# Experts' raw weights loaded into the place of their low part, and two places for a tile's inner rows

## What is computed

```python
def _moe2_ref(x, w_gate, w_output_gate, w1, w2) -> np.ndarray:
    logits = x @ w_gate
    e_idx = np.argmax(logits, axis=1)
    ...
    for e in range(E):
        mask = e_idx == e
        ...
        h = np.maximum(x[mask] @ w1[e], 0.0)
        ye = h @ w2[e]
        out[mask] = gate_w[mask, None] * eom[mask, e, None] * ye
```

## Time and profile before

| | |
|---|---|
| median of three runs | 1172.2 us (1169.95, 1172.2, 1597.25) |
| the profiled execution | 1167.76 us, its span 1166.0 us |
| mean granted TensorE clock | 0.988 |
| TensorE matmuls busy | 1127.7 us, 97% of the span |
| VectorE, ScalarE, GpSimd busy | 639.4, 466.8, 76.8 us |
| DMA over the span | 131.36 MB, mean 113 GB/s |

### The profile page before, as it was taken

The page is one execution under the profiler, slowest core; times in us unless marked ns, Lnnn a source line. Parts: engine busy times, 40 slices in busy tenths (PEclk is TensorE's granted clock), DMA queues, the critical chain, the costliest instruction groups (busy, mean ns, idle before and its releaser), DMA issues.

```text
span 1166.0 us, 20895 instructions
## 1 busy us (share of the span) xinstructions
PE 1127.7 (97%) x6358; PEld 886.0 (76%) x6359; DVE 639.4 (55%) x1247; ACT 466.8 (40%) x780; POOL 76.8 (7%) x96
## 2 busy tenths in 40 slices
PE   9999999999999999999999988989999999979995
PEld 7777777777777777777778977777888888858884
DVE  6675654655646556556564347557464435556632
ACT  4554434443444444434544351435342223344420
POOL 0000100101001001010010110010011010100000
PEclk9999999999999999999999989999999999989998
DMA  9210110101001100110020275677675444856442
GB/s 375 80 37 10 64 37 37 40 34 74 37 1 73 37 37 37 37 73 1 1 109 1 79 258 182 205 274 228 191 261 169 146 144 128 284 161 208 156 140 63
DMA packets 98783, 131.36 MB, mean 113 GB/s; under 512 B 13967, under 2 KB 75023, under 8 KB 94352
## 3 DMA queue, kind: packets, MB, share of 16 engines
q1 hardware_dynamic: 91360, 89.35, 23.7%
q10 hardware_dynamic: 1584, 23.07, 5.5%
q0 software_dynamic: 5760, 17.90, 4.0%
HBM read 85.86 MB, written 45.47 MB: 113 GB/s over the span
## 4 chain that ended last, share of the span: by engine, by line
PE 85%; DVE 4%; issue 3%; DMA 2%; SPq 2%; ACTq 2%; ACT 1%; DVEq 0%; POOL 0%; POOLq 0%
PE y_ps L855 33%; PE h_ps L837 15%; PE y_ps L928 13%; PE y_ps L912 7%; PE h_ps L912 6%; PE a_ps L812 2%; PE h_ps L827 2%; DMA hid_mv<-hidden 1%; ACTq L444 1%; DVE we L483 1%; PE a_ps L715 1%; PE a_ps L796 1%; PE a_ps L776 1%; DMA hidden<-expert_hid 1%; SPq L574 1%
## 5 line engine op out<-in xcount | busy, mean ns | idle before, releaser
L855 PE MATMUL y_ps<-w_out_hi,hid_hi 128*128 128x512 f32 x544 | 218.6, 402 | 0.0
L855 PE MATMUL y_ps<-w_out_lo,hid_hi 128*128 128x512 f32 x544 | 213.0, 392 | 0.0
L855 PE MATMUL y_ps<-w_out_hi,hid_lo 128*128 128x512 f32 x544 | 212.6, 391 | 0.0
L928 PE MATMUL y_ps<-we,act_t_hi 128*128 (+1 forms) x608 | 187.9, 390 | 4.4 <-issue 2.6
L1365 DVE SCALAR_TENSOR_TENSOR hid<-hid,h_ps 128x512 f32<-128x512 f32 (+1 forms) x144 | 94.4, 656 | 168.2 <-ACT hid L1035 168.2
L837 PE MATMUL h_ps<-att_hi,mix 128*128 128x512 f32 x512 | 184.5, 403 | 0.1
L1035 ACT ACTIVATE hid<-h_ps,three 128x512 f32<-128x512 f32 (+1 forms) x144 | 95.4, 662 | 177.4 <-PE h_ps L837 154.0
L855 PEld LDWEIGHTS y_ps<-w_out_hi,hid_hi 128*128 128x128 f32 x544 | 102.1, 188 | 51.1 <-issue 30.4
L928 PEld LDWEIGHTS y_ps<-we,act_t_hi 128*128 128x128 f32 x608 | 113.9, 188 | 30.3 <-issue 6.1
L1374 DVE TENSOR_TENSOR hid_lo<-hid,hid_hi 128x512 fp32r<-128x512 f32 (+1 forms) x144 | 94.8, 658 | 70.5 <-ACT hid_hi L1043 70.0
L1552 DVE STREAM_TRANSPOSE act_raw<-hid_mv 128x512 f32<-128x512 f32 x76 | 49.5, 690 | 132.7 <-DMA hid_mv<-hidden 131.3
(11 more groups left out here) (216 smaller groups left out, 1410.9 us busy)
## 6 DMA issues: line engine op xcount, KB each, us to landing
raw<-in_w ACTq DMA_DIRECT2D x11, 2048.0 KB, 8.4
hidden<-expert_hid SPq DMA_DIRECT2D x76, 256.0 KB
hid_mv<-hidden SPq DMA_DIRECT2D x152, 128.0 KB, 2.9
xg<-buckets SPq DMA_DIRECT2D x164, 64.0 KB, 1.9
xb<-in_x_rows SPq DMA_DIRECT2D x8, 1024.0 KB, 4.9
x_t<-in_x_t SPq DMA_DIRECT2D x7, 1024.0 KB, 5.0
buckets<-pad_row SPq DMA_DIRECT2D x8, 774.0 KB, 8.5
raw<-in_w SPq DMA_DIRECT2D x3, 2048.0 KB, 8.1
```

What stands on the lines that cost most here:

```text
L855: i = pe.matmul(y_ps[:, t, :], (hid_hi, hid_lo)[hp][:, hid_at(b, j), t * P:(t + 1) * P], w_out_s[wp][:, j, :], start=(j == 0 and m == 0), ...
L928: i = pe.matmul(y2_ps[:, slot % 2, :], act_t[hp][:, slot % 2, f, :], we[:, bass.ds(w_at + (wp * WPART + KD * F + f * DM), DM)], start=(f = ...
```

## The change

- `raw1`, `raw2` are left for the first expert alone. All other raw weights are loaded into `we_raw`, which is the low part's place in the slot to be filled (the slots' order becomes high 0, low 0, low 1, high 1), and split in place: VectorE reads raw there and writes low over it.
- A load can thus not start before the slot is free. T_LOAD now holds in an expert's first tile: at the start of ScalarE's body, before relu, w1 of the next expert is loaded, when `first` of tile t-1 is done. T_SPLIT holds in an expert's second tile, or in its first if it has only one: w1 is split behind `hidden_hi(t-1)`, and right behind it w2 of the next expert is loaded, when `second` of the old expert's last tile is done (y2_ps at T_FIRST). w2 is split in the tile two after the one with T_SPLIT, as the last step of the body. VectorE splits in the same order, w1 before w2.
- `raw1`'s place is given to a second `expert_hid` and a second `hid_mv`. Relu waits for the write of tile t-2 instead of t-1, and the move back waits for the turn of tile t-2 instead of t-1.
- SyncE moves inner rows back before it loads the gate. It no longer loads the second expert's w1; with it go two VectorE steps and a copy of the table, and another step is added.

```diff
-    WSLOT = 2 * (KD * F + KE * DM)
     WPART = KD * F + KE * DM
...
-    we = at("we", 0, [P, 2 * WSLOT], F32R)
+    we = at("we", 0, [P, 4 * WPART], F32R)
+    we_raw = at("we_raw", WPART * 4, [P, 2 * WPART], F32)
...
-    expert_hid = at("expert_hid", late_at, [P, F], F32)
+    expert_hid = [at(f"expert_hid{i}", o, [P, F], F32) for i, o in enumerate((late_at, raw1_at))]
+    hid_mv = [at(f"hid_mv{i}", o, [P, 2, STRIPS, P], F32)
+              for i, o in enumerate((163840 + 2 * STRIPS * P * 4, raw1_at + F * 4))]
...
+    def part_at(w_at, part):
+        return w_at * 3 if part == HI else w_at + WPART
...
-        sp.wait_ge(sem("second_ready"), 1)
-        e = sp.value_load(table[0:1, T_NEXT, MT:MT + 1], min_val=0, max_val=E - 1)
-        sp.wait_ge(sem("w1_ready"), 1)
-        sp.dma_start(raw1[:], w1[bass.ds(e, 1)].rearrange("o p k f -> p (o k f)")).then_inc(sem("raw1_loaded"), 16)
...
             if not (isinstance(t.n, int) and t.n + 3 >= MT):
                 load_rows(t.plus(3))
+            wait(sp, "hid_written", 16 * HALVES * (t.n + 1))
+            if not (t.first or is_b(t.n, 1)):
+                wait(sp, "hid_turned", HALVES * (t.n - 1))
+            for j in range(STRIPS):
+                sp.dma_start(hid_mv[place][NS * j:NS * j + NS, :, :, :],
...
             load_gate(t)
-            wait(sp, "hid_written", 16 * HALVES * (t.n + 1))
-            wait(sp, "hid_turned", HALVES * t.n)
-            for j in range(STRIPS):
-                sp.dma_start(hid_mv[NS * j:NS * j + NS, :, :, :],
...
+        def load_weights(w, raw_dram, e, w_at, *free):
+            size = (KD * F, KE * DM)[w]
+            for slot, is_there in ((0, w_at < 1), (WPART, w_at > 0)):
+                with act.If(is_there):
+                    at_raw = piece(w, 0, slot)
+                    for there in free:
+                        wait(act, *there)
+                    act.dma_start(we_raw[:, at_raw:at_raw + size], raw_dram[bass.ds(e, 1)].rearrange("o p k f -> p (o k f)")
+                                  ).then_inc(sem(f"raw{w + 1}_loaded"), 16)
 
         def body(t):
             if not t.last:
                 rows_hi(t.plus(1))
+            load = entry(act, t, T_LOAD)
             split1 = entry(act, t, T_SPLIT)
-            if not t.first:
-                split2 = entry(act, t.plus(-1), T_SPLIT)
+            if not (t.first or is_b(t.n, 1)):
+                split2 = entry(act, t.plus(-2), T_SPLIT)
+            with act.If(load > 0):
+                e = entry(act, t, T_NEXT, E - 1)
+                other = entry(act, t, T_OTHER, WPART)
+                load_weights(0, w1, e, other, ("y_ps", CH * B + ST) if t.first else ("hid2_ps", HALVES * t.n))
             for h in range(HALVES):
                 wait(act, "hid2_ps", HALVES * t.n + h + 1)
-                if h == 0:
-                    wait(act, "hid_written", 16 * HALVES * t.n)
+                if h == 0 and not (t.first or is_b(t.n, 1)):
+                    wait(act, "hid_written", 16 * HALVES * (t.n - 1))
...
             if not t.first:
                 hidden_hi(t.plus(-1))
-                if is_b(t.n, 1):
-                    load_w2(entry(act, Tile(0, MT), T_NEXT, E - 1), 1)
-                before_it = t.plus(-1)
-                with act.If(split2 > 0):
...
+            with act.If(split1 > 0):
+                n = entry(act, t, T_ORD, E - 1) + 1
+                e = entry(act, t, T_NEXT, E - 1)
+                other = entry(act, t, T_OTHER, WPART)
+                first_tile = entry(act, t, T_FIRST, MT)
+                split_hi(0, n, other)
+                load_weights(1, w2, e, other, *(() if t.first else (("y2_ps", first_tile),)))
+            if not (t.first or is_b(t.n, 1)):
+                before_it = t.plus(-2)
+                with act.If(split2 > 0):
+                    n = entry(act, before_it, T_ORD, E - 1) + 1
+                    other = entry(act, before_it, T_OTHER, WPART)
                     split_hi(1, n, other)
...
-        chain(dve.scalar_tensor_tensor(out=second_of[:], in0=nth[:], scalar=2.0, in1=used_no[:],
-                                       op0=ALU.is_equal, op1=ALU.mult))
-        chain(dve.tensor_reduce(second[:], second_of[:], AX.X, ALU.add))
-        dve.tensor_copy(table[:, T_NEXT, MT:MT + 1], second[:]).then_inc(sem("second_ready"), 1)
...
-        chain(dve.scalar_tensor_tensor(out=t_chg[:], in0=t_pos[:], scalar=2.0, in1=t_chg[:],
+        chain(dve.scalar_tensor_tensor(out=t_chg[:], in0=t_pos[:], scalar=1.0, in1=t_chg[:],
                                        op0=ALU.is_lt, op1=ALU.mult))
-        chain(dve.scalar_tensor_tensor(out=t_chg[:], in0=t_pos[:], scalar=2.0, in1=t_chg[:],
+        chain(dve.scalar_tensor_tensor(out=t_chg[:], in0=t_pos[:], scalar=1.0, in1=t_chg[:],
                                        op0=ALU.is_equal, op1=ALU.add))
...
+        chain(dve.tensor_scalar(t_chg[:], t_pos[:], 1.0, None, ALU.is_lt))
```

More of the change, by code:

```diff
@@ L1102, in rows_hi @@
                            ).then_inc(sem("xg_t_hi"), 1)
-        split_hi(1, 0, 0)
+        split_hi(1, 0, 0, raw=raw2)
         rows_hi(Tile(0, 0))
@@ L1158, in body @@
-                    if not is_b(t.n, 1):
-                        wait(act, "y2_ps", first_tile)
-                    split_hi(1, n, other)
-                    with act.If(load > 0):
-                        load_w2(e, n + 1)
-            with act.If(split1 > 0):
-                n = entry(act, t, T_ORD, E - 1) + 1
-                other = entry(act, t, T_OTHER, WSLOT)
-                wait(act, "hid2_ps", HALVES * t.n)
-                split_hi(0, n, other)
+                    other = entry(act, before_it, T_OTHER, WPART)
@@ L1546, in turn_hidden @@
             slot = t.slot
-            wait(dve, "hid_moved", 16 * STRIPS * (t.n + 1))
+            wait(dve, f"hid_moved{slot % 2}", 16 * STRIPS * (t.u * (RING // 2) + t.c // 2 + 1))
             if not (t.first or is_b(t.n, 1)):
@@ L1566, in body @@
             if t.first:
-                split_lo(dve, 1, 0, 0, range(1, PIECES), "w2_ready")
+                split_lo(dve, 1, 0, 0, range(1, PIECES), "w2_ready", raw2)
             if not (isinstance(t.n, int) and t.n < 3):
@@ L1570, in body @@
             split1 = entry(dve, t, T_SPLIT)
+            if not (t.first or is_b(t.n, 1)):
+                split2 = entry(dve, t.plus(-2), T_SPLIT)
             if not t.first:
-                split2 = entry(dve, t.plus(-1), T_SPLIT)
                 turn_hidden(t.plus(-1))
@@ L1577, in body @@
                 hidden_lo(t.plus(-1))
[L1578 removed]
+            with dve.If(split1 > 0):
+                split_lo(dve, 0, entry(dve, t, T_ORD, E - 1) + 1, entry(dve, t, T_OTHER, WPART), signal="w1_ready")
+            if not (t.first or is_b(t.n, 1)):
+                before_it = t.plus(-2)
                 with dve.If(split2 > 0):
[L1580 removed]
+                    split_lo(dve, 1, entry(dve, before_it, T_ORD, E - 1) + 1, entry(dve, before_it, T_OTHER, WPART),
                              signal="w2_ready")
[L1582 to L1583 removed]
         def finish(t):
```

87 lines of the change are left out of this document (32 added, 55 removed).

## The result

| | median | span of the profiled execution | TensorE's granted clock |
|---|---|---|---|
| before | 1171.1 us (4 runs) | 1166.0 us | 0.988 |
| after | 1198.7 us (4 runs) | 1195.5 us | 0.975 |

The change makes the kernel 2.4% slower: ratio 1.0242, 95% interval 1.0217 to 1.0268; one execution of before that took 1597.25 us is left out of the ratio. The medians are 27.6 apart: the profiled execution of before is one of its fastest.

The account below looks back on a forecast made before the run. TensorE, busy 97% of the span, was taken as the bound, so only its waits could pay. 1167.8 + 7.4 (start) + 21.5 (tiles 27 to 30) - 1.0 (end) = 1195.7, put at 1198 for a median; range 1176 to 1207.

Parts of the forecast that it names:

- Start: First tiles: w1's load ahead of relu 0 delays inner rows; new stalls 15.3 against 7.6 and 0.3 saved, +7.4 us.
- The table's 0.3: Table before the tiles: loses three small VectorE steps and gains one, so 0.3 us earlier.
- the rival, a write that lands as if the load weren't there: Loads and writes take turns, in all tiles: +10.6 us, 1182 by the median; chance 0.18.
- Tile 29: Start of tile 29: ScalarE waits for tile 26's last `second` before loading w2; stall 2.4 us.
- `second` of tile 28: TensorE wants w2's split at 19.1 us after tile 26's `second` ends, gets it at 36.3: stall 17.2 us.
- E+36.3: E is the end of `second` of tile 26; w2's split was to reach TensorE 36.3 us after it.
- C: Tiles 27 to 30, around an expert of one tile: 2.4 + 17.2 + 1.9 for the lower clock = +21.5 us.
- End: Last tile: gate's load behind the moves shortens TensorE's 2.6 us wait for inner rows, -1.0 us.
- "25 of 1167.8 can be won.": Last stage: TensorE's waits, 21 us, plus some 4 at the lower clock are all that can be won, 2.1%.
- A: The working for the start, first tiles, +7.4 us; it gives ScalarE's split of w1 3.9 us.
- the worse rival: Late ScalarE runs into further loads, every term at its upper bound: 1204.4, 1209 by the median, or more; chance 0.09.
- that of the start alone: Only the start costs, nothing at tiles 27 to 30 because tile 27 was misread: 1172.2 + 6.4 = 1179; chance 0.10.

Follow-up runs that it names:

- the two runs without the hold before tile 29: Changed kernel with one load at a register's address instead of two branched loads: 1199.2 us, 1.0249; changed kernel with five tiles instead of four ahead of the loops: 1196.4 us, 1.0222.
- Two edits without any change of memory: Kernel before, with the gate loaded behind the moves and w1 split ahead of relu (ScalarE) and of the turn (VectorE): 1151.6 us, 0.9831.

## Why the forecast held, and where it was off

- **Forecast** 1198 (1176 to 1207), measured 1198.7. The sum was 1195.7 for the profiled execution, which took 1197.2. None of the rivals came. That the total is so close is in part luck: the terms below are off by -1.8, +3.1 and +0.3.
- **Start, +7.4 forecast, 5.6 measured.** Two terms hold: `second` of tile 0 waits 6.1 (6.6), tile 3 2.2 (2.4). The stalls of 2.4 at `second` of tile 4 and 2.0 at tile 7 didn't come; in their place stand 0.5 at tile 7 and 1.2 at `second` of 5. ScalarE was some 2 us sooner with w1's second load (767.8 instead of 770.0). The table's 0.3 does not show: the first `first` starts 0.85 later, but over all runs here it starts anywhere from 707.8 to 709.9, with the change or without.
- **A transfer behind a load lands 1 to 2 us after the load.** Right: the writes of 721.5 and 1058.2 land at 729.5 and 1066.3, 1.0 us after the loads of 719.96 and 1056.38, which take 8.5 and 8.9 us. So the rival, a write that lands as if the load weren't there, did not come.
- **Regular experts, 0.** Right, and one place for inner rows is no worse.
- **Tile 28, 7.6 taken as it was:** 6.5.
- **Tile 29, 2.4 forecast, 8.3 measured.** This is the step that failed: the sum counted ScalarE's registers and branches in time but not in code. The longer loop is fetched anew, behind the load just issued, and the rows of tile 29 come 6.6 us behind it instead of 1.0.
- **`second` of tile 28, stall 17.2 forecast, 12.3 measured.** E+36.3 became E+40.1, since everything behind the fetch was 4 to 5 us late (from the turn of tile 28's inner rows to TensorE it took the 15.1 us forecast), and TensorE itself came 9 us later (8.3 instead of 2.4 before tile 29, and more time at the lower clock). The two errors nearly cancelled by luck, which the two runs without the hold before tile 29 show: there this stall is 16.3 and 15.1, and the time is the same. The mechanism was right and its size was fixed by the chain from E, not by the single waits.
- **The clock, 1.9 forecast in C.** The waits of C rose by 19.5 (8.3 + 12.3 - 1.1), the stretch by 24.6: some 5 us are the lower clock, behind three waits instead of one. This term was mis-sized by 3.
- **End, -1.0 forecast:** -1.8, with 1.1 more behind the last `second`.
- **"25 of 1167.8 can be won."** Two edits without any change of memory took 19.7. For these the missing place for inner rows and raw weights wasn't what the waits stood on; the order of steps was.
- **Two slips of the working, without effect.** C prices the split of w1 at 2.9 where A has 3.9. And the forecast adds 2.3 to its sum for a median, while the worse rival and that of the start alone add 4.4.

## What to carry to other kernels

A buffer that is loaded only when its last reader is done ties the load, its flight, the split and everything queued behind on the issuing engine to that reader: ask how short the shortest case is (here an expert of one tile), not only whether the regular case has slack. Before giving memory to a wait, see whether a step that is already ready can stand ahead of one that still waits. And count the instructions of an engine's loop: some twenty more to a tile, never executed, cost 7.5 us here.

## What the hardware showed that was not expected

- ScalarE's loop of four tiles shows no packets on the instruction queue in 300 us at 76 instructions a tile, 2 at some 83, and 31 to 34 at 89 and more (counts as given ahead of the runs). With the longer loop in the kernel before, its 33 packets cost TensorE one long wait. Behind a 2 MB load issued just before the jump ScalarE is held for 5 to 6 us more (6.4 and 6.6 instead of 1.0).
- A wait of TensorE of 1.8 us can be followed by products at a mean clock of 0.77, and one of 2.6 us by products at 1.00.
